# Four input sets, a second set of moved blocks and a second running-sum bank in an attention, expert and feed-forward kernel

## The reference

```python
k_sum = k.reshape(B, H, nb, block, D).max(axis=3)
v_sum = v.reshape(B, H, nb, block, D).mean(axis=3)
scores_l = scale * np.matmul(q, k.transpose(0, 1, 3, 2))      # masked to |i - j| < 16
scores_s = scale * np.einsum('bhsd,bhnd->bhsn', q, k_sum) + np.log(block)
```

## Time and profile before

| what | value |
|---|---|
| median of 3 runs | 900.49 us (898.7 to 901.21) |
| profiled execution, its own time | 899.4 us |
| its span | 897.6 us |
| PE busy | 834.9 us, 93% |
| DVE / ACT / POOL busy | 559.8 / 409.7 / 536.2 us |
| DMA read and written | 70.73 MB, 3.17 MB |
| mean granted TensorE clock | 0.97 of full speed |

### The profile page before, as it was taken

One profiled execution on the slowest core, in us unless ns is written; L12 is line 12 of the kernel. 1 busy time (PEld: TensorE's weight loads), 2 busy tenths in 40 slices (PEclk: granted clock), 3 DMA queues, 4 the chain that ended last, 5 costly groups with the idle time before them and its releaser, 6 DMA issues.

```text
span 897.6 us, 13871 instructions
## 1 busy us (share of the span) xinstructions
PE 834.9 (93%) x5008; PEld 811.5 (90%) x5008; DVE 559.8 (62%) x1204; ACT 409.7 (46%) x906; POOL 536.2 (60%) x400
## 2 busy tenths in 40 slices
PE   5475999999999999899999999998999997999998
PEld 4364999999999999899999999997999997999998
DVE  3475575676656657766666565657565657565565
ACT  3385445454454434433333343345454555455451
POOL 1186565556646678665656556589566489556550
PEclk9676999999999999999999999999999999999999
DMA  9662143321521221121312212121112121312101
GB/s 247 166 170 83 65 126 129 98 74 68 162 71 48 77 83 48 65 94 48 113 48 80 80 50 92 48 95 47 48 55 87 47 92 50 115 50 95 48 1 71
DMA packets 26420, 74.79 MB, mean 83 GB/s; under 512 B 14704, under 2 KB 15728, under 8 KB 20208
## 3 DMA queue, kind: packets, MB, share of 16 engines
q1 hardware_dynamic: 26352, 73.90, 25.5%
HBM read 70.73 MB, written 3.17 MB: 82 GB/s over the span
## 4 chain that ended last, share of the span: by engine, by line
PE 68%; DVE 10%; issue 7%; POOL 7%; DMA 4%; ACT 3%; SPq 1%; DVEq 0%; POOLq 0%; ACTq 0%
PE bank L953 22%; PE bank L955 21%; PE bank L954 21%; DMA k_win<-k_w 2%; POOL t_late L471 2%; PE bank L906 2%; DVE xa L774 2%; DVE bank L811 2%; DVE h_lo L817 2%; POOL wu_lo L446 2%; DVE xb_lo L763 2%; PE bank L945 1%; PE bank L919 1%; DMA v_cols<-v_t 1%; DVE snap L787 1%
## 5 line engine op out<-in xcount | busy, mean ns | idle before, releaser
L774 DVE TENSOR_TENSOR xa<-bank,xa 128x384 f32<-128x384 f32 x352 | 195.7, 556 | 233.6 <-PE bank L955 229.6
L953 PE MATMUL bank<-xb_hi,wu_hi 128*128 128x384 f32 x672 | 233.2, 347 | 26.9 <-DVE h_lo L817 13.6
L953 PE MATMUL bank<-h_hi,wd_hi 128*128 128x384 f32 x768 | 257.9, 336 | 0.1
L955 PE MATMUL bank<-h_lo,wd_hi 128*128 128x384 f32 x768 | 257.5, 335 | 0.0
L954 PE MATMUL bank<-h_hi,wd_lo 128*128 128x384 f32 x768 | 257.4, 335 | 0.0
L608 ACT ACTIVATE h_hi<-bank 128x384 fp32r<-128x384 f32 x192 | 94.5, 492 | 296.7 <-DVE bank L807 244.3
L954 PE MATMUL bank<-xb_hi,wu_lo 128*128 128x384 f32 x672 | 227.2, 338 | 0.0
L955 PE MATMUL bank<-xb_lo,wu_hi 128*128 128x384 f32 x672 | 227.1, 338 | 0.0
L452 POOL TENSOR_TENSOR wd_lo<-stage,wd_hi 128x1024 fp32r<-128x1024 f32 x48 | 115.5, 2407 | 182.6 <-ACT wd_hi L582 182.6
L953 PEld LDWEIGHTS bank<-xb_hi,wu_hi 128*128 128x128 f32 x672 | 127.9, 190 | 36.7 <-issue 27.8
L446 POOL TENSOR_TENSOR wu_lo<-w_sum,wu_hi 128x1024 fp32r<-128x1024 f32 x48 | 115.2, 2399 | 56.0 <-ACT wu_hi L576 56.0
(11 more groups left out here) (59 smaller groups left out, 828.6 us busy)
## 6 DMA issues: line engine op xcount, KB each, us to landing
stage<-weights SPq DMA_DIRECT2D x48, 1024.0 KB, 4.9
k_win<-k_w SPq DMA_DIRECT2D x8, 720.0 KB, 6.3
v_win<-v_w SPq DMA_DIRECT2D x8, 576.0 KB, 5.1
q_bd<-q_t SPq DMA_DIRECT2D x16, 192.0 KB, 7.0
v_cols<-v_t SPq DMA_DIRECT2D x8, 384.0 KB, 6.7
p_bc<-p_rows SPq DMA_DIRECT2D x8, 384.0 KB, 5.7
out<-xa SPq DMA_DIRECT2D x4, 384.0 KB, 7.5
out<-xa SPq DMA_DIRECT2D x8, 192.0 KB, 1.9
```

The lines of the kernel that those rows point to most:

```text
L774: nc.vector.tensor_tensor(at, y_bank(g, t), at, ALU.add).then_inc(y_taken, 1)
L953: nc.tensor.matmul(dst, w_h, a_h, start=first, stop=False, skip_group_check=True)
L955: return nc.tensor.matmul(dst, w_h, a_l, start=False, stop=last, skip_group_check=True)
```

## The change

It does six things.

1. Four input sets (`SETS = 4`): all four units of the first sequence have their own; the second sequence uses two of them in turn. The order of SP's loads changes with that (stage 1's weights later, two units of the second sequence ahead of step 0).
2. Keys in rows (`k_raw`, 768 columns and 16 of padding at each side) in place of windows. The copy of the maxima on POOL goes; `scores` issues two matmuls for each tile in its place, one over 96 keys and one over the 24 maxima, each with the same stationary queries. The first group of a unit waits for `kmax_done` itself.
3. The mean of the values goes to a small tile on ACT (24 x 128, with the factor 1/32), and POOL copies it twelve times into `v_win` (`spread_value_means`, 24 x 1536). The turns of the value sums on PE move from the first step of a unit, behind P6, to the second step of the unit before it, behind P7, and into bank 5.
4. A second set of moved blocks (`xb_other`, phases 1 and 3) in the memory of attention. A phase's seven blocks are made in the last three steps of the phase before, `part` 0, 1, 2; all low parts of phases 1 to 3 are made on DVE, and two buffers (`t_early`, `t_late`) hold the sums instead of four.
5. Two banks for the running sum: odd steps after 13 use bank 7, so that P1 waits for C21 of the step before the last.
6. POOL sums the weights in another order, a21 + a22 in place in the stage; four blocks are now raw and three are sums (`RAW = 4 * BW`), `high_raw` waits for POOL's second sum and `high_sums` is one instruction. In the first sequence each fourth copy of the transposes goes to ACT.

```diff
-        with ExitStack() as early:
-            q_bd = [None, sb(early, "q_bd1", [P, TILES, P])]
-            k_win = [None, sb(early, "k_win1", [P, TILES, KEYS])]
+            for i in (2, 3):
+                input_set(early, i)
...
+        xb_other = moved_blocks(ctx, "xb_other", NP)
+        t_late = sb(ctx, "t_late", [P, 2, 2, HALF])
...
+        def preparing(g):
+            return next(((ph + 1, g - LAST[ph] + 2) for ph in range(3) if 0 <= LAST[ph] - g < 3), (None, None))
+        def two_banks(g):
+            return g > ATT_OVER and g % 2 == 1
+        def ps_x(g):
+            return bank[7 if two_banks(g) else 0][:, 0:HALF]
...  # POOL, one step
+                if part == 0:
+                    sum_moved(ph, 1)
+                if part == 1:
+                    sum_moved(ph, 3)
                 if g + 1 < STEPS:
                     low_sums(g + 1)
-                if g in LAST[:3]:
-                    low_moved(ph + 1, 2)
+                for u in turned(g):
+                    spread_value_means(u, sumlo_done, g + 2)
+                if part == 0:
+                    sum_moved(ph, 2)
+                if part == 1:
+                    sum_moved(ph, 4)
                 if g + 1 < STEPS:
                     low_down(g + 1)
...  # ACT, one step
                 keep(g, 1)
                 if more:
-                    high_sums(g + 1, 1)
+                    high_sums(g + 1)
+                if part is not None:
+                    high_moved(ph, (0, 3, 4)[part])
                 keep(g, 2)
...
                     high_down(g + 1, 0)
                     high_down(g + 1, 1)
+                if part is not None:
+                    high_moved(ph, (1, 6, 5)[part])
                 if ffn:
                     sigmoid(g, "C12")
                 high_hidden(g, "C12")
+                if part == 0:
+                    high_moved(ph, 2)
...  # DVE, one step
                     take_y(g - 1, 4)
+                if part is not None:
+                    low_moved(ph, (0, 3, 4)[part])
                 add_c22(g)
...
                 low_hidden(g, "C22")
                 low_hidden(g, "C21")
+                if part is not None:
+                    low_moved(ph, (1, 6, 5)[part])
                 add_c12(g)
                 if g:
                     take_y(g - 1, 7)
                 gate(g, "C12")
+                if part == 0:
+                    low_moved(ph, 2)
+                for u in unit_after(g, 0):
+                    value_sums(u)
+                for u in unit_after(g, 1):
+                    key_maxima(u)
...  # DVE, between attention of the first sequence and step 0
+            low_moved(0, 1)
+            sum_first(2)
+            low_moved(0, 3)
+            low_moved(0, 6)
+            sum_first(4)
+            low_moved(0, 5)
+            value_sums(KT)
             key_maxima(KT)
...  # PE
                 for t in range(GT):
-                    last = nc.tensor.matmul(s_bank(k)[:, t * KEYS:(t + 1) * KEYS], q_bd[at_set(u)][:, t0 + t, :],
-                                            k_win[at_set(u)][:, t0 + t, :], start=True, stop=True)
+                    nc.tensor.matmul(at[:, 0:KW], query, k_raw[at_set(u)][:, QT * (t0 + t):QT * (t0 + t) + KW],
+                                     start=True, stop=True)
+                    last = nc.tensor.matmul(at[:, KW:KEYS], query, k_max[:, u % 2, :], start=True, stop=True)
...
-                    wait_count(pe, hlo_done, 4 * (g - 1) + READY["C21"])
+                    if two_banks(g) and not two_banks(g - 2):
+                        pe.wait_ge(x_done, ALL_GROUPS)
+                    else:
+                        before = g - 2 if g > ATT_OVER + 2 else g - 1
+                        wait_count(pe, hlo_done, 4 * before + READY["C21"])
```

More of the change, by code:

```diff
@@ L55 @@
 BW = 2 * P
-RAW = 3 * BW
+RAW = 4 * BW
 UPW = NP * BW
@@ L87, in constants, with attention_moe_ffn @@
     return c
-def attention_moe_ffn(nc, consts, q_t, k_w, v_t, v_w, probs, weights, p_rows, out):
+def attention_moe_ffn(nc, consts, q_t, k_t, v_t, v_w, probs, weights, p_rows, out):
     ctx = ExitStack()
@@ L237, in v_bank @@
         def v_bank(u):
[L238 to L245, removed]
+            return bank[2] if u < KT else bank[5]
         def columns(k):
@@ L290, in y_bank, with hidden, ungated @@
             return bank[banks[t % len(banks)]][:, 0:HALF]
[L292 to L309, removed]
+        def two_banks(g):
+            return g > ATT_OVER and g % 2 == 1
+        def ps_x(g):
+            return bank[7 if two_banks(g) else 0][:, 0:HALF]
+        def hidden(g, c):
+            return {"C11": ps_y, "C22": ps_y, "C12": ps_z}.get(c, ps_x(g))
+        def ungated(g, c):
+            return snap[:, 2, :] if c == "C22" else hidden(g, c)
         @block.sync
@@ L589, in keep @@
                     act.wait_ge(c_done, 3 * (g - 1) + (1, 3, 2)[n])
-                nc.scalar.activation(snap[:, n, :], ps_x, ACT.Copy).then_inc(snap_done, 1)
+                nc.scalar.activation(snap[:, n, :], ps_x(g), ACT.Copy).then_inc(snap_done, 1)
             def sigmoid(g, c):
-                at = {"C11": ps_y, "C22": snap[:, 2, :], "C21": ps_x, "C12": ps_z}[c]
                 n = READY[c]
@@ L600, in sigmoid @@
                 wait_count(act, gated_done, 4 * g + n - 2)
-                nc.scalar.activation(sig[:, n % 2, :], at, ACT.Sigmoid, scale=1.702).then_inc(sig_done, 1)
+                nc.scalar.activation(sig[:, n % 2, :], ungated(g, c), ACT.Sigmoid, scale=1.702).then_inc(sig_done, 1)
             def high_hidden(g, c):
-                at = {"C11": ps_y, "C22": ps_y, "C21": ps_x, "C12": ps_z}[c]
                 act.wait_ge(gated_done, 4 * g + READY[c])
                 wait_count(act, y_done, 8 * (g - 1))
-                nc.scalar.activation(h_hi[:, g % 2, TILE[c], :], at, ACT.Copy).then_inc(hhi_done, 1)
+                nc.scalar.activation(h_hi[:, g % 2, TILE[c], :], hidden(g, c), ACT.Copy).then_inc(hhi_done, 1)
             for slot in range(SLOTS):
@@ L796, in gate @@
                 n = READY[c]
-                at = {"C11": ps_y, "C22": ps_y, "C21": ps_x, "C12": ps_z}[c]
-                of = {"C22": snap[:, 2, :]}.get(c, at)
                 if c == "C21":
@@ L810, in gate @@
                     dve.wait_ge(sig_done, 4 * (g - FFN0) + n)
-                    nc.vector.tensor_tensor(at, of, sig[:, n % 2, :], ALU.mult).then_inc(gated_done, 1)
+                    nc.vector.tensor_tensor(hidden(g, c), ungated(g, c), sig[:, n % 2, :], ALU.mult
+                                            ).then_inc(gated_done, 1)
             def low_hidden(g, c):
-                at = {"C11": ps_y, "C22": ps_y, "C21": ps_x, "C12": ps_z}[c]
                 dve.wait_ge(hhi_done, 4 * g + READY[c])
-                nc.vector.tensor_tensor(h_lo[:, g % 2, TILE[c], :], at, h_hi[:, g % 2, TILE[c], :].bitcast(F32),
-                                        ALU.subtract).then_inc(hlo_done, 1)
-            for s in range(2):
+                nc.vector.tensor_tensor(h_lo[:, g % 2, TILE[c], :], hidden(g, c),
+                                        h_hi[:, g % 2, TILE[c], :].bitcast(F32), ALU.subtract).then_inc(hlo_done, 1)
+            for s in range(SETS):
                 nc.vector.memset(q_bd[s][DH:P, :, 0:DH], 0.0).then_inc(q_zeroed_low, 1)
```

441 lines of the change are left out of this document (226 added, 215 removed).

## The result

The changed kernel takes 932.16 us (median of 4 runs, 930.74 to 933.10) against 899.60 us (898.28 to 901.21, 4 runs): a ratio of 1.036 with the interval 1.0336 to 1.0384. It is slower by 32 us, and outside the range that was forecast. The profiled execution's span is 930.2 us against 897.6, 32.6 more.

| piece | before | after | difference | forecast |
|---|---|---|---|---|
| A, up to step 1's first snap copy | 94.9 | 105.8 | +10.9 | -11.4 |
| its last output copy ends at | 69.1 | 78.2 | +9.1 | -13.1 |
| B, steps 1 to 12 | 216.8 | 224.1 | +7.3 | +6.1 |
| C, steps 13 to 46 | 560.3 | 575.2 | +14.9 | +9.1 |
| tail | 25.5 | 25.1 | -0.5 | 0 |

What follows compares the result with a forecast made beforehand. PE, busy 93% of the span, was taken as the bound, with waits at the start and phase changes. From 899.4 us: A -11.4, B +6.1, C +9.1 gave 903.2 us, range 867 to 913.

Steps and rivals of the forecast that it cites:

- A: Start, up to step 1's first snap copy: first sequence ends 13.1 us earlier, step 0 takes 1.7 more; -11.4 us (-19 to -2).
- B: Attention, steps 1 to 12: doubled score matmuls +8.9 us, first steps of units -2.8; sum +6.1 us (-3 to +9).
- C: Steps 13 to 46: second bank -5.1 us, phase changes 39 us in place of 24.8 (+14.2); sum +9.1 us.
- tail: Step 47, at the end of the kernel: untouched by the change, 0 us.
- PE's idle time in the slots covers it: First sequence: 16 score matmuls a group instead of 8, 0.8 us more at full clock, hidden in PE's idle time.
- Rival 1: Phase changes: DVE's slack in three steps absorbs the seven low parts, refill hides; C -27 us, time 867; chance 0.20.
- Rival 3: Start: loads bound it, last output copy stays near 69 us; A +2 us, time 917; chance 0.08.
- Rival 2: Phase changes: low parts do not queue behind POOL, each costs 0.95 us; C -10 us, time 884; chance 0.18.
- rival 4: Attention steps: 24-column matmuls nearly free, the rest as forecast; B -1.7 us, time 895; chance 0.10.

## Why the prediction was wrong, by its own steps

**A, the start: the step that failed.** "PE's idle time in the slots covers it", for 0.8 us a group. That weighed the added matmuls at the full clock and left the clock out, though the kernel before already ran this stretch at a mean clock of 0.71:

```profile
20.40:69.10 48.70, 29.75 (x303) 24.61 (x303) 27.23 (x113) 27.61 (x98) 25.21 (x23) 0.71 0.69 175
```

The 19 us in which PE stands there are the idle time that was counted on. With the added matmuls PE ran the first sequence at the half clock up to 72.3 us. There a slot of a group is about 5.5 us of PE: 3.4 for scores (four tiles at 0.85), 1.0 for transposes, 1.1 for values. PE was the bound, from which no idle time could cover anything, and the end of the sequence came at 78.2 instead of 56. Most of that is the clock: with as many matmuls, the second one wide, the end is at 61.6 and 60.5. The 4 to 5 us from there to the 56.9 of one matmul per tile come with the second matmuls even so: the idle time did not cover them whole. That 56.9 lies near the forecast 56 is luck in part, since the forecast had two matmuls in it.

Step 0 took 105.8 - 78.2 = 27.6 us against 27.5 forecast: right. The loads, for which I had widened A, did not bind: in the kernel with one matmul per tile no engine waits for a load between 20 and 57 us. POOL set the pace there, as forecast, in so far as PE waits 8.8 us for its normalizations. Its copies took 1.46 us each (2 forecast); whether they have a part in that wait was not tested.

That the 24-column matmuls are behind the half clock is shown from both sides. The five kernels with them rise to the full clock at 70.4 to 78.0 us (the changed one, the kernel before with split scores, and the three that rearrange C alone). With 96 columns, with 120, or with one matmul they first rise at 10.4 to 17.9, the kernel before at 20.4 and at 18.9 with two banks. What in these matmuls the chip goes by is not settled: the kernel with 120 columns also has another order of the two, and the one with 96 moves keys in place of maxima.

**B, the attention steps: right.** 18.71 - 17.78 = 0.93 us a group (0.8 forecast), and 0.90 with 96 or 120 columns in the second matmul: the columns cost nothing, the number of matmuls does. The Trainium skill's rule ("TensorE: Matmul & The Clock Gate", section LDWEIGHTS, 107 ns for 128 stationary columns, whatever moves) is borne out nearly: (0.93 us)/8 is 0.116 us. Its floor of 25 ns for a gap is not what sets this pair. The turning steps lost as much as forecast: 19.62, 19.27 and 19.23 us for steps 1, 4 and 7 against 18.71, which is 0.9, 0.6 and 0.5 us (0.5 forecast).

**C, the phase changes: the mechanism right, a size off.** Plain steps 16.06 to 15.60: right. PE stands for 29.6 us in steps 13 to 46 (575.2 less 545.6 busy) against 34 of stalls forecast, for the reasons given: P5 released by low C12, 4.55 us late after part 0 and 2.43 and 1.49 after parts 1 and 2 of the same change. Taking away ACT's lateness, or POOL's turn, or both with the third block, brought C's excess to 14.4, 28.2 and 4.1. The term that was mis-sized is the clock's: 27.3 us at the half clock are 13.6 lost if each gives half (an estimate), against 5 forecast. I had given a clock drop to the three longest stalls; the trace has six, behind stands of 2.43 to 4.96 us, and two of them last 6.8 us.

The price of one drop was misread, too. The forecast read 1.7 us lost behind the stand of step 15. The kernel before with split scores has the same stand of 2.59 us there and no half clock behind it, and the stretch from that stand to the end of the next is as long. The windows of the kernel before and of the one with split scores (columns as above):

```profile
361.40:367.90 6.50, 6.00 (x25) 5.71 (x25) 5.21 (x8) 2.34 (x4) 6.42 (x6) 0.74 0.43 161
```

```profile
386.00:392.50 6.50, 4.42 (x25) 4.12 (x25) 5.21 (x8) 2.34 (x4) 6.42 (x6) 1.00 0.45 161
```

At the full clock PE only reaches its next wait earlier. C's excess is 29.7 us there without any half clock, and 29.9 in the kernel before with 10.2 us of it. In the changed kernel such a drop does cost something: step 14 has 3.4 us less of it in the kernel with one matmul per tile and takes 21.35 us instead of 22.41. So 13.6 is an upper bound.

**The rivals.** None of the four happened. Rival 1 (the refill hides) is true of the kernels with all low parts moved: 4.1 and 2.1 us are left, where it had 3. It failed here for the reason given against it, the order on DVE. Rival 3 (the start does not move, by the loads) had the sign of A, but not the cause: the loads did not bind with one matmul. Rival 2 fails by the low part of 2.51 us beside POOL, rival 4 by the 0.93 us a group. The worst start in any case of mine was rival 3's, 2 us later than before; it is 10.9 later, so that neither the range nor a chance held the result.

## What to carry to other kernels

Where a change makes matmuls more numerous and shorter, price them at the clock that they will get, and look at the places where PE has idle time: there the price may be double, and the idle time gone. Check the pace by the spacing of equal instructions, not by the clock column, where a trace has no clock record yet. Time at the half clock is lost only as far as PE would not have had to wait at the end of it anyway. And when one wait is taken out of a chain, follow it to the next bank that the same late instruction frees: two banks alone gave back all that they gained.

## What the runs showed of the hardware

- More work for PE made a kernel faster: 192 matmuls of 120 columns, 96 of them zeros, in place of 24-column ones took 17.5 us off (891.03 to 873.52), in a kernel that also has a smaller DMA scratch.
- A tile's two matmuls took 0.85 us under a shown clock of 1.00, where the same two take 0.45 later: before the trace's first clock record the column shows full speed.
- The half clock behind a stand is not always as long: 3.4 us behind each of the three stands of 2.55 to 2.59 us in the kernel before, 6.8 behind each of the three of 3.14 to 4.00 us in the kernel with two banks alone, and none behind the same three stands in the kernel before with split scores, whose steps 13 to 46 take as long (560.1 us for 560.3).
- DVE's and POOL's instructions with two inputs in SBUF again finished one behind the other: a low part of 0.95 us alone took 2.51 beside POOL's.
